# Row maxima chunk by chunk, division on gathered sums, and a differently divided opening in a fused attention and feed-forward kernel

## The reference

```python
q_pool = q.reshape(B, H, S // 2, 2, D).mean(axis=3)          # 576 pooled queries per head
scores = (1 / sqrt(D)) * np.matmul(q_pool, k.transpose(0, 1, 3, 2))
scores = scores - np.max(scores, axis=-1, keepdims=True)
attn = np.exp(scores)
attn = attn / (np.sum(attn, axis=-1, keepdims=True) + 1e-09)
o = np.matmul(attn, v)                                       # 16 heads x 576 x 64
x = o.transpose(0, 2, 1, 3).reshape(1152, 512)
h = x @ w_in;   x = (h * np.tanh(softplus(h))) @ w_out       # first feed-forward layer
h = x @ w_in2;  x = np.where(h > 0, h, exp(min(h, 0)) - 1) @ w_out2
```

## Time and profile before

| | |
|---|---|
| median of 3 runs | 705.26 us (703.49 to 706.42) |
| profiled execution | 703.71 us |
| its span | 701.9 us |
| TensorE busy | 657.8 us, 94% |
| VectorE, ScalarE, GpSimd busy | 423.4, 397.0, 426.5 us |
| DMA | 54.30 MB, mean 77 GB/s |

### The profile page before, as it was taken

One profiled execution on the slowest core, in us unless ns is written; L12 is line 12 of the kernel. 1 busy time (PEld: TensorE's weight loads), 2 busy tenths in 40 slices (PEclk: granted clock), 3 DMA queues, 4 the chain that ended last, 5 costly groups with the idle time before them and its releaser, 6 DMA issues.

```text
span 701.9 us, 12236 instructions
## 1 busy us (share of the span) xinstructions
PE 657.8 (94%) x3984; PEld 636.7 (91%) x3984; DVE 423.4 (60%) x620; ACT 397.0 (57%) x743; POOL 426.5 (61%) x388
## 2 busy tenths in 40 slices
PE   3589999999999999999999999999999999999997
PEld 2478889898898988899999999999999999999997
DVE  6667878787887876377777665777543332223222
ACT  2357888888888878755555555555643322222221
POOL 4266788888888866587786666787644422222221
PEclk9599999999999999999999999999999999999999
DMA  5355564555556540012220000122222110001001
GB/s 162 96 155 157 147 174 135 163 159 158 143 147 163 157 110 16 16 50 71 62 61 0 0 0 30 48 67 67 60 77 61 46 45 0 0 0 46 1 1 45
DMA packets 31503, 54.30 MB, mean 77 GB/s; under 512 B 4752, under 2 KB 10208, under 8 KB 31456
## 3 DMA queue, kind: packets, MB, share of 16 engines
q1 hardware_dynamic: 31296, 53.66, 27.7%
q10 hardware_dynamic: 160, 0.04, 0.0%
HBM read 30.93 MB, written 2.36 MB: 47 GB/s over the span
## 4 chain that ended last, share of the span: by engine, by line
PE 67%; POOL 8%; ACT 8%; DVE 7%; issue 7%; DMA 2%; SPq 1%; POOLq 0%; ACTq 0%; DVEq 0%
PE py L490 9%; PE py L491 8%; PE py L492 8%; PE pH L475 8%; PE pH L476 8%; PE pH L477 8%; PE pm L398 5%; DVE part_max L712 3%; PE po L430 3%; PE po L431 3%; PE po L432 3%; PE ps L413 3%; PE ps L414 3%; POOL pl L931 3%; ACT ph L565 2%
## 5 line engine op out<-in xcount | busy, mean ns | idle before, releaser
L986 POOL TENSOR_TENSOR gl<-fg,gh 128x384 fp32r<-128x384 f32 x96 | 97.3, 1014 | 142.4 <-ACT gh L655 141.1
L931 POOL TENSOR_TENSOR pl<-p,ph 128x576 fp32r<-128x576 f32 x72 | 106.0, 1480 | 67.4 <-ACT p L571 63.3
L712 DVE TENSOR_REDUCE part_max<-pm 128x2 f32<-128x768 f32 (+1 forms) x123 | 111.1, 904 | 39.9 <-PE pm L398 38.1
L490 PE MATMUL py<-gh,wout_h 128*128 128x384 f32 x384 | 129.2, 336 | 3.6 <-DVE xl L842 2.2
L491 PE MATMUL py<-gl,wout_h 128*128 128x384 f32 x384 | 128.4, 334 | 0.0
L492 PE MATMUL py<-gh,wout_l 128*128 128x384 f32 x384 | 128.3, 334 | 0.0
L477 PE MATMUL pH<-xh,win_l 128*128 (+1 forms) x384 | 128.3, 334 | 0.0
L475 PE MATMUL pH<-xh,win_h 128*128 (+1 forms) x384 | 128.3, 334 | 0.0
L476 PE MATMUL pH<-xl,win_h 128*128 (+1 forms) x384 | 128.3, 334 | 0.0
L565 ACT ACTIVATE ph<-ps 128x576 fp32r<-128x576 f32 x144 | 93.9, 652 | 51.2 <-PE ps L414 48.8
L821 DVE RECIPROCAL fi<-fp 128x192 f32<-128x192 f32 x48 | 64.9, 1353 | 52.2 <-POOL fp L994 52.1
(11 more groups left out here) (68 smaller groups left out, 1367.7 us busy)
## 6 DMA issues: line engine op xcount, KB each, us to landing
kh<-k_hi SPq DMA_DIRECT2D x60, 144.0 KB, 2.6
w_raw<-w_in SPq DMA_DIRECT2D x32, 256.0 KB, 2.7
w_raw<-w_out SPq DMA_DIRECT2D x32, 256.0 KB, 2.6
k_pack<-kP SPq DMA_DIRECT2D x16, 288.0 KB, 3.2
q_raw<-qT SPq DMA_DIRECT2D x16, 288.0 KB, 3.1
v_raw<-v SPq DMA_DIRECT2D x16, 288.0 KB, 2.9
kl<-k_pack SPq DMA_DIRECT2D x32, 144.0 KB, 2.4
q<-q SPq DMA_DIRECT2D x16, 144.0 KB, 2.5
```

The source lines that it names most:

```text
L490: pe.matmul(out, hi, gh[:, f % 4, :], start=(f == 0), stop=False)
L712: dve.tensor_reduce(part_max[:, par, 2 * g:2 * g + wide], group_banks(n, g)[:, 0:wide, 0:MC], AX.X, ALU.max).then_inc(m_read, 1)
L931: pool.tensor_tensor(pl[:, ph_slot(slot, kt), :], p32[:, p32_slot(n, kt) % 3, :], ph[:, ph_slot(slot, kt), :].bitcast(F32), ALU.subtract). ...
```

## The change

- *Chunks.* Behind head 0, `max_chunk` replaces `max_group`: one chunk of 384 keys, one bank of `pm`, one semaphore step, one VectorE instruction. The tables give for each tile how many chunks stand ahead of PV and how many behind it. VectorE's program is now led by the chunks: `SPLIT_BEHIND` names the chunk behind which each subtraction stands.
- *Tiles.* `POOL_KT` gives GpSimd the odd tiles, and scores always stand ahead of PV.
- *Division.* ScalarE copies all of `po` at once, at the start of the next head. SyncE gathers the 576 sums of a head from one row onto 64 partitions x 9 columns, VectorE adds 1e-9 and inverts 9 columns for a pair of heads, SyncE gathers the inverses back into one row for each head and then copies that row to 63 more partitions (`gather_inv`, `spread_inv`); it also moves the odd head's output (`move_o`). VectorE multiplies once.
- *Rows of maxima* are sent by SyncE.
- *Opening.* q is loaded before k. VectorE sums it and makes `q1`; ScalarE makes three of the four quarters of head 0's `kh` and writes the row of -1; GpSimd writes the constants of `vt` and of the second buffers; seven chunks of head 1 stand before head 0's first PV, four of them before its first scores.

```diff
-POOL_KT = ((2, 4, 5, 6, 8), (2, 4, 5, 8))
+POOL_KT = ((1, 3, 5, 7, 8), (1, 3, 5, 7))
...
-FIRST_GROUPS = (2, 2, 2, 2, 0, 1, 1, 1, 2)
-GROUPS = (1, 1, 1, 0, 1, 1, 1, 1, 1)
+EARLY_CHUNKS = (4, 3)
+FIRST_CHUNKS = ((2, 1), (1, 1), (1, 1), (1, 0), (1, 1), (1, 1), (1, 1), (1, 1), (1, 1))
+CHUNKS = ((1, 0), (2, 0), (2, 0), (0, 0), (2, 0), (1, 1), (2, 0), (1, 1), (1, 1))
+FIRST_SPLIT_BEHIND = {5: (1, 0), 8: (1, 2), 11: (1, 4), 14: (1, 6)}
+SPLIT_BEHIND = {3: (2, 8), 5: (1, 0), 8: (1, 2), 12: (1, 4), 14: (1, 6)}
+INVERT_BEHIND, FINALIZE_BEHIND = 14, 6
...
+            def spread_row(m):
+                par = m % 2
+                sp.wait_ge(q2_preset[par], 1)
+                sp.wait_ge(max_ready, m + 1)
+                sp.dma_start(q2[par][D:D + 1, :].bitcast(F32).rearrange("o (t c) -> o t c", c=P),
+                             row_turned[0:QT, par, :]).then_inc(row_spread, 16)
+            def gather_sums(m):
+                par, pair = m % 2, m // 2
+                sp.wait_ge(o_copied, m + 1)
+                wait(sp, sum_kept, pair)
+                source = D * (1 - par)
+                sp.dma_start(sum_few[par * D:par * D + D, :],
+                             o_rows[source:source + 1, par, :].rearrange("o (r c) -> o r c", c=FEW)).then_inc(sums_in[par], 16)
+            def move_o(p):
+                sp.wait_ge(o_copied, 2 * (p + 1))
+                sp.wait_ge(sums_in[0], 16 * (p + 1))
+                sp.dma_start(o_rows[D:2 * D, 0, :], o_rows[D:2 * D, 1, :]).then_inc(o_moved, 16)
+            def gather_inv(p):
+                sp.wait_ge(sum_inv, p + 1)
+                wait(sp, x_ready, p)
+                for par in range(2):
+                    sp.dma_start(inv_wide[par * D:par * D + 1, :].rearrange("o (r c) -> o r c", c=FEW),
+                                 inv_few[par * D:par * D + D, :]).then_inc(inv_in, 16)
+            def spread_inv(p):
+                sp.wait_ge(inv_in, 32 * (p + 1))
+                for par in range(2):
+                    first = par * D
+                    sp.dma_start(inv_wide[first + 1:first + D, :],
+                                 inv_wide[first:first + 1, :].unsqueeze(1).to_broadcast([1, D - 1, SQ])).then_inc(inv_spread, 16)
...
+            load_q(0)
             load_kp(0)
-            load_q(0)
             load_kp(1)
             load_v(0)
             next_q(1)
+            spread_q2(0)
             spread_kl(0)
-            spread_q2(0)
-            next_q(2)
             spread_kh(1)
             spread_q1(1)
+            next_q(2)
+            spread_row(0)
             load_kp(2)
             spread_kl(1)
             spread_q2(1)
...
             for n in range(HEADS):
...
                 if n + 1 < HEADS:
                     load_w(w_in[0][n + 1], 0, n + 1, (n + 1) % 2)
+                if n % 2 == 0 and n > 0:
+                    gather_sums(n - 1)
+                    move_o(n // 2 - 1)
+                elif n % 2:
+                    gather_sums(n - 1)
+                if n + 1 < HEADS:
+                    spread_row(n + 1)
+                if n % 2 == 0 and n > 0:
+                    gather_inv(n // 2 - 1)
                 if n + 2 < HEADS:
                     spread_kl(n + 2)
                     spread_q2(n + 2)
+                if n % 2 == 0 and n > 0:
+                    spread_inv(n // 2 - 1)
+                if n + 2 < HEADS:
+                    load_v(n + 2)
                 if n + 3 < HEADS:
                     spread_kh(n + 3)
                     spread_q1(n + 3)
                 if n + 4 < HEADS:
                     next_q(n + 4)
                     load_kp(n + 4)
+            gather_sums(HEADS - 1)
+            move_o(PAIRS - 1)
+            gather_inv(PAIRS - 1)
+            spread_inv(PAIRS - 1)
...
+            def max_chunk(n, j):
+                at, (t, c) = chunk_count(n, j), divmod(j, 3)
+                if j == 0:
                     pe.wait_ge(kh_spread, 64 * (n + 1))
                     pe.wait_ge(q1_spread, 64 * (n + 1))
...
+                wait(pe, m_read, at - 1)
+                pe.matmul(pm[:, at % 2, 0:MC], q1[:, n % 3, t * P:t * P + P], kh[n % 3][:, c * MC:c * MC + MC],
+                          start=True, stop=True).then_inc(m_filled, 1)
...
+            pe.wait_ge(first_read, NG)
...
+            for j in range(EARLY_CHUNKS[0]):
+                max_chunk(1, j)
+            for kt in range(AHEAD - 1):
                 scores(0, kt)
+            for j in range(EARLY_CHUNKS[0], sum(EARLY_CHUNKS)):
+                max_chunk(1, j)
+            scores(0, AHEAD - 1)
...
                 for kt in range(KT):
...
                     nxt = ahead(n, kt)
...
+                    if nxt is not None:
                         scores(*nxt)
...
+                    for head, j in chunks_at(n, kt, 0):
+                        max_chunk(head, j)
+                    pv(n, kt)
+                    for head, j in chunks_at(n, kt, 1):
+                        max_chunk(head, j)
...
             def copy_o(n):
                 act.wait_ge(pv_done, KT * (n + 1))
...
+                if n % 2 == 0:
+                    wait(act, x_ready, n // 2)
+                else:
+                    wait(act, o_moved, 16 * (n // 2))
+                    wait(act, sums_in[1], 16 * (n // 2))
+                act.activation(halves(o_rows[:, n % 2, :]), po[:, :, 0:HQ], ACT.Copy).then_inc(o_copied, 1)
...
+            preset_sign(0)
+            act.wait_ge(q_summed, 1)
+            act.activation(q_hi[:, :], q_sum[:, :], ACT.Copy).then_inc(first_rounded, 1)
             round_k(0)
+            first_keys(slice(D, 2 * D), slice(0, HK), slice(0, D))
+            first_keys(slice(D, 2 * D), slice(HK, SK), slice(D, 2 * D))
+            first_keys(slice(0, D), slice(HK, SK), slice(D, 2 * D))
+            round_k(1)
+            split_q(1)
             split_v(0)
-            split_q(1)
-            round_k(1)
-            spread_row(0)
+            preset_sign(1)
+            split_q(2)
...
+            def max_chunk(n, j):
+                at, par = chunk_count(n, j), n % 2
+                dve.wait_ge(m_filled, at + 1)
+                dve.tensor_reduce(part_max[:, par, j:j + 1], pm[:, at % 2, 0:MC], AX.X, ALU.max).then_inc(m_read, 1)
+                if j == NCH - 1:
+                    dve.wait_ge(m_read, at + 1)
+                    turn_row(n)
...
+            def invert(p):
+                dve.wait_ge(sums_in[0], 16 * (p + 1))
+                dve.wait_ge(sums_in[1], 16 * (p + 1))
+                dve.tensor_scalar(sum_few[:, :], sum_few[:, :], 1e-9, None, ALU.add).then_inc(sum_kept, 1)
+                dve.wait_ge(sum_kept, p + 1)
+                wait(dve, inv_in, 32 * p)
+                dve.reciprocal(inv_few[:, :], sum_few[:, :]).then_inc(sum_inv, 1)
+            def finalize(p):
+                dve.wait_ge(inv_spread, 32 * (p + 1))
+                dve.wait_ge(o_moved, 16 * (p + 1))
                 wait(dve, xl_done, p)
...
-            def finalize(p):
...
+            dve.memset(kl[0][D:2 * D, :].bitcast(F32), 0.0).then_inc(kl_preset[0], 1)
+            dve.memset(q2[0][D:2 * D, :].bitcast(F32), 0.0).then_inc(q2_preset[0], 1)
+            dve.wait_ge(q_in, 16)
+            dve.tensor_tensor(q_sum[:, :], q_raw[:, 0, :], q_raw[:, 1, :], ALU.add).then_inc(q_summed, 1)
+            dve.wait_ge(first_rounded, 1)
+            for part, cols in ((slice(0, D), slice(0, HQ)), (slice(D, 2 * D), slice(HQ, SQ))):
+                dve.tensor_copy(q1[D:2 * D, 0, cols], q_hi[part, :].bitcast(F32)).then_inc(q1_spread, 16)
+                dve.tensor_tensor(q1[0:D, 0, cols], q_sum[part, :], q_hi[part, :].bitcast(F32),
+                                  ALU.subtract).then_inc(q1_spread, 16)
             dve.wait_ge(k_rounded, 1)
...
+            dve.tensor_copy(kh[0][0:D, 0:HK], k_hi[0:D, :].bitcast(F32)).then_inc(kh_spread, 16)
...
+            for m in range(1, HEADS + 2):
+                for j in range(NCH):
+                    if m < HEADS:
+                        max_chunk(m, j)
+                    if j == INVERT_BEHIND and m % 2 and 3 <= m < HEADS:
+                        invert((m - 3) // 2)
+                    if j == FINALIZE_BEHIND and m % 2 == 0 and 4 <= m <= HEADS:
+                        finalize((m - 4) // 2)
+                    if j in (SPLIT_BEHIND if m > 1 else FIRST_SPLIT_BEHIND):
+                        back, kt = (SPLIT_BEHIND if m > 1 else FIRST_SPLIT_BEHIND)[j]
+                        if 0 <= m - back < HEADS and kt in VKT[(m - back) % 2]:
+                            split_p(m - back, kt)
+            invert(PAIRS - 1)
...
+            preset_v(0)
+            pool.memset(kl[1][:, :].bitcast(F32), 0.0).then_inc(kl_preset[1], 1)
+            pool.memset(q2[1][:, :].bitcast(F32), 0.0).then_inc(q2_preset[1], 1)
+            pool.wait_ge(q1_spread, 64)
             split_k(0)
             sum_q(1)
             split_q(1)
+            split_k(1)
             split_v(0)
-            split_k(1)
+            preset_v(1)
```

(2 more changed lines are left out.)

259 lines of the change are left out of this document (89 added, 170 removed).

## The result

The changed kernel takes **763.48 us** (median of 4 runs, 761.71 to 764.27) against 705.15 us before (4 runs on the same chip): a ratio of 1.0825, 95% interval 1.0796 to 1.0855. It is 8.2% slower; the forecast was 686 us, range 676 to 699.

What follows compares the result with a forecast made beforehand. TensorE, busy 94%, bounds the kernel and loses time waiting for VectorE's maxima reads; 701.9 - 10.2 (opening) - 15.0 (heads 1 to 13) + 5 (last division) = 681.7, with profile-to-median offsets 685.1, stated as 686 us, range 676 to 699.

Steps and rivals of the forecast that it cites:

- part (3) of the long stage: VectorE at `finalize`, heads 1 to 13: broadcasts land at 13.5, VectorE stands 0.9 us, TensorE loses 0.6 a pair.
- Rival C: SyncE's queue: broadcasts behind `kl` land late, VectorE stands with chunks behind it; 4 us late gives 713 us; chance 0.09.
- The last division: Between last PV and first output matmul: division loses its cover, output matmul 5.1 us later; +5, bounds +4.5 and +9.
- The opening: Up to PV(1): earlier start and chunk-by-chunk maxima bring it to 45.8 from 56.0; -10.2, bounds -3.7 and -13.
- Rival D: The opening gives only its start, head 0 being held by the clock and split order; 691.6 us; chance 0.08.
- rival A: The maxima handshake stays in heads 1 to 13, 15.8 us a head; 695 us; chance 0.17.
- The long stage: Heads 1 to 13: 15.0 us a head, 195.6 instead of 210.6; -15.0, bounds -20.8 and -5.2.
- the stand of VectorE at `finalize`: Once per pair in heads 1 to 13: VectorE waits 0.9 us for the broadcasts, costing TensorE 0.6 a pair.
- the handshake: TensorE and VectorE over maxima banks: one chunk per bank removes waiting, 1.74 us of each 16.2 us head.
- the copy: At a head's start, PV waits for ScalarE's copy of `po`: 0.15 wait plus 0.1 restart, 0.25 us a head.
- Small operations on VectorE: New addition and reciprocal of 9 columns for the division: 0.15 us each, bounds zero and 1.05 us.

Runs made afterwards that it cites:

- e1: Changed kernel, each broadcast row read from a partition of its own instead of all 63 from one (inverses not delivered): 706.94 us, ratio 1.0032.
- e2: Changed kernel, each broadcast writes 64 rows instead of 63, over 16 engines instead of 9, still from one source partition: 761.38 us, ratio 1.0811.
- e7: Changed kernel, broadcasts of 288 columns instead of 576 from the second pair on (the other inverses not spread): 725.79 us, ratio 1.0318.
- e4: Changed kernel, a pair's inverses written to DRAM and spread from there to 64 rows per half: 696.65 us, ratio 0.9898.
- e13: e9 with SyncE issuing the gather of the sums and the move of the odd head's output ahead of the weight load: 682.12 us, ratio 0.97.
- e6: e4 with the spread of the inverses issued ahead of the kl and q2 moves: 686.59 us, ratio 0.9764.
- e8: Kernel before the change, with only the maxima handed over chunk by chunk from head 1 on: 699.09 us, ratio 0.9939.
- e12: Changed kernel with the old division put back, without its second copy at the head's start from head 2 on: 684.29 us, ratio 0.9726.
- e9: e6 with VectorE's final product of the last pair moved behind the first feed-forward unit's division: 686.19 us, ratio 0.9745.
- e15: Changed kernel, still broadcasting from one SBUF partition, with the spread issued ahead of the kl and q2 moves: 760.86 us, ratio 1.0817.

## Why the prediction was wrong

**The failed step** is in part (3) of the long stage: "The broadcasts are issued 10.5 to 11.7 and land at 13.5, 2.4 behind the last issue". The 2.4 us were `kl`'s, 144 KB read from as many partitions as it writes. By size it was the nearest row. But no row of the trace before had many reads of one partition, and I gave that landing no upper bound, where for other unseen costs I took two. It landed 10.8 us behind. Four runs show that the source is the cause: e1 changes it alone and the loss is gone, e2 excludes the number of engines, e7 shows that bytes count, and e4 takes another route. One thing stays open: all these packets read the same 2304 bytes, and no run tells many reads of one partition from many reads of one address in it.

**Rival C** had the mechanism, its place and its sign, with a chance of 0.09. Its price, a microsecond for each that VectorE stands, holds: the seven stands in the heads are 9.0 us on average instead of 0.9, 57 on 685, so 742. The last division adds 8. The lower clock, which the price left out, adds 17: behind each of these stands TensorE works 4.3 to 5.7 us at 1.2 GHz and loses half of that. Less the 3 us of the opening that makes 764, against 763 measured. But the forecast put the lateness down to SyncE's queue ("The broadcasts stand in order behind `kl`"). The last issue was 1.0 us late of the 9.4; the rest is the transfer. And it set the number of engines aside as a matter of tenths, which e2 bears out. The rule that bore on it stands on another page of the Trainium skill, "SBUF — State Buffer", in the section on the DMA port swizzle: bandwidth goes by how many of 16 ports the partitions reach, 27 GB/s each. The runs agree in kind, with 32 to 35 GB/s from one partition.

**The opening** was right in kind and at its far bound: PV(1) at 42.9, 13.1 us earlier, forecast 10.2. The first maxima matmuls come at 7.62 (forecast 8.0), the first score at 18.35 (20.1), PV(0) at 25.6 (26.6). Rival D is out. So is rival A: head 1 took 15.3 us after, not 15.8, and TensorE hardly waits for maxima in e13.

**The long stage.** With the landing mended, 195.6 us were forecast for heads 1 to 13 (thirteen heads of its 15.0 us are 195.1); e4 took 215.2, e6 205.6, e13 199.5. Two steps were mis-sized. First, the stand of VectorE at `finalize` was taken as 0.9 us and 0.6 us of TensorE a pair; in e4 it stood 1.6 to 2.5 us, even heads took 16.7 to 18.3 us, and the odd head behind three of them 16.2 to 16.7 at a clock of 0.90 to 0.93. Second, the handshake: by itself it gives 1.7 us over 13 heads (e8), and the rest comes only together with the new placing and the new division. The forecast named the copy as a cost of 0.25 us and never saw that, with this placing, a second copy would have cost 0.8 us a head (e12). That e6 stands at 686.6, the forecast's own number, is luck, errors that nearly cancel: 10 us more in heads 1 to 13, against 2.9 less in the opening, 1.9 in heads 14 and 15 and 1.1 each in the last two stretches.

**The last division** was forecast at 16.7 us behind the last PV, against 11.6. In the changed kernel it is 24.6, and with the spread from DRAM 15.6 to 16.5 (e4, e9, e13). The term of +5 was right once the landing is.

The chance of 0.07 for slower was too small, with a transfer that no row had measured in the path of every pair.

## What to carry to other kernels

A transfer is priced by where it reads as much as by its bytes: a spread out of one SBUF partition ran at 32 GB/s here and held up what was queued behind it, and the same rows out of DRAM or of partitions of their own ran four times as fast and more. When the trace has no row for an access pattern, its price has no upper bound yet; measure it alone, or put it where a few microseconds more harm nobody. And a wait that stops TensorE for long can be paid twice, once as idle time and again at the lower clock behind it: 9 us and 2.5 us a pair here, and nothing of the second in e13, whose waits are tenths.

## What the runs showed of the hardware

- Many packets that read the same row of one SBUF partition share 32 to 35 GB/s. With next to no other traffic (head 14), 126 packets of 2304 bytes took 9.2 us, 128 on more engines 9.0 (e2), 126 of 1152 bytes 4.1 (e7), and 126 of 2304 bytes from partitions of their own 2.3 (e1).
- Through DRAM, 4.5 KB written and spread again to 128 rows landed in 1.6 and 3.2 us (e4), although the 64 rows of a half read the same 2304 bytes.
- A slow broadcast holds up SyncE's later issues, not only its own landing: four issues of `kh` took 6.0 us instead of 2.4 (2.4 to 2.8 in e1), two of `kl` 7.8 instead of 1.1 (e15).
- Small operations on VectorE, estimated at 0.15 us each, took 0.17 us at best for the addition of 9 columns (0.36 on average of eight, 0.69 at most) and 0.22 for their reciprocal.
